# Retention attention and two feed-forward blocks on one core: another form of the warming products, and fewer waits on TensorE in the attention

## The reference

```python
# q, k, v: (4, 8, 768, 64)
for t in range(S):                       # attention with a decaying state
    state = gamma[None, :, None, None] * state + np.einsum('bhd,bhe->bhde', k[:, :, t], v[:, :, t])
    y[:, :, t] = scale * np.einsum('bhd,bhde->bhe', q[:, :, t], state)
...
x = y as (3072, 512)
h = x @ w_in                             # 512 -> 2048
g = np.where(h > 0.0, h, np.exp(np.minimum(h, 0.0)) - 1.0)
x = g @ w_out                            # 2048 -> 512
...
h = x @ w_in2                            # 512 -> 1024
solu = h * softmax(h)
ln = (solu - mean) / sqrt(var + 1e-6) * g_ln
out = ln @ w_out2                        # 1024 -> 512
```

## Time and profile before

| | |
|---|---|
| time, median of 3 runs | 837.15 us (837.04 to 837.56) |
| the profiled execution | 837.55 us, its span 835.8 us |
| TensorE busy | 831.1 us (99% of the span), 4861 product records |
| VectorE, ScalarE, GpSimd busy | 559.2, 412.8, 398.9 us |
| the warming | 13 products from 1.19 us |
| first scores product | 6.50 us |
| first product behind the attention (line 685) | 75.25 us |

### The profile page before, as it was taken

The page is one execution under the profiler, slowest core; times in us unless marked ns, Lnnn a source line. Parts: engine busy times, 40 slices in busy tenths (PEclk is TensorE's granted clock), DMA queues, the critical chain, the costliest instruction groups (busy, mean ns, idle before and its releaser), DMA issues.

```text
span 835.8 us, 12629 instructions
## 1 busy us (share of the span) xinstructions
PE 831.1 (99%) x4861; PEld 692.5 (83%) x4861; DVE 559.2 (67%) x854; ACT 412.8 (49%) x660; POOL 398.9 (48%) x460
## 2 busy tenths in 40 slices
PE   9999999999999999999999999999999999999998
PEld 7998888888888888888888888888888888888886
DVE  5587767678634555575455555788877778777774
ACT  3685766574435555553455555563333343334422
POOL 3797857754026574620267661564334444444200
PEclk9999999999999999999999999999999999999999
DMA  9999312105012010140201001612111111111001
GB/s 351 404 397 320 102 51 69 58 26 177 1 39 63 26 51 26 52 150 1 75 26 51 27 26 54 198 51 76 51 51 51 51 50 39 51 52 51 17 21 51
DMA packets 48651, 72.79 MB, mean 87 GB/s; under 512 B 2896, under 2 KB 23504, under 8 KB 48336
## 3 DMA queue, kind: packets, MB, share of 16 engines
q1 hardware_dynamic: 48448, 71.84, 24.9%
q10 hardware_dynamic: 144, 0.15, 0.1%
HBM read 55.20 MB, written 16.78 MB: 86 GB/s over the span
## 4 chain that ended last, share of the span: by engine, by line
PE 99%; ACT 0%; issue 0%; DVE 0%; ACTq 0%
PE ps L733 10%; PE ps L736 10%; PE ps L732 10%; PE ps L685 9%; PE ps L687 9%; PE ps L686 9%; PE ps L856 5%; PE ps L854 5%; PE ps L855 5%; PE ps L744 5%; PE ps L746 5%; PE ps L745 5%; PE ps L611 3%; PE ps L654 3%; PE ps L840 3%; PE ps L630 1%
## 5 line engine op out<-in xcount | busy, mean ns | idle before, releaser
L523 POOL TENSOR_TENSOR u_lo<-u_raw,u_hi 128x256 fp32r<-128x256 f32 x168 | 141.5, 875 | 192.8 <-ACT u_hi L1250 192.8
L733 PE MATMUL ps<-g_hi,wd_lo 128*128 128x512 f32 x384 | 149.4, 389 | 0.0
L732 PE MATMUL ps<-g_hi,wd_hi 128*128 128x512 f32 x384 | 149.4, 389 | 0.0
L736 PE MATMUL ps<-g_lo,wd_hi 128*128 128x512 f32 x384 | 149.4, 389 | 0.0
L685 PE MATMUL ps<-x_hi,u_hi 128*128 128x512 f32 x336 | 131.3, 391 | 0.0
L687 PE MATMUL ps<-x_lo,u_hi 128*128 128x512 f32 x336 | 130.8, 389 | 0.0
L686 PE MATMUL ps<-x_hi,u_lo 128*128 128x512 f32 x336 | 130.7, 389 | 0.0
L518 POOL TENSOR_TENSOR u_raw<-u_raw 128x256 f32<-128x256 f32 x96 | 88.8, 926 | 16.2 <-DMA u_raw<-w_dram 10.3
L568 POOL TENSOR_TENSOR u_lo<-x_raw,u_hi 128x256 fp32r<-128x256 f32 x84 | 65.5, 814 | 41.8 <-ACT u_hi L1373 41.8
L732 PEld LDWEIGHTS ps<-g_hi,wd_hi 128*128 128x128 f32 x384 | 72.1, 188 | 15.1
L733 PEld LDWEIGHTS ps<-g_hi,wd_lo 128*128 128x128 f32 x384 | 72.1, 188 | 15.0
(11 more groups left out here) (94 smaller groups left out, 1450.4 us busy)
## 6 DMA issues: line engine op xcount, KB each, us to landing
u_raw<-w_dram SPq DMA_DIRECT2D x24, 512.0 KB, 3.5
q<-units_dram SPq DMA_DIRECT2D x12, 512.0 KB, 6.8
k<-units_dram SPq DMA_DIRECT2D x12, 512.0 KB, 8.2
v<-units_dram SPq DMA_DIRECT2D x12, 512.0 KB, 7.9
x_between<-x SPq DMA_DIRECT2D x24, 256.0 KB, 2.8
x_raw<-x_between SPq DMA_DIRECT2D x12, 512.0 KB, 3.6
out_dram<-y_sb SPq DMA_DIRECT2D x24, 256.0 KB, 2.0
kn<-units_dram SPq DMA_DIRECT2D x9, 512.0 KB, 9.7
```

The source lines that it names most:

```text
L523: nc.gpsimd.tensor_tensor(u_lo[n % 2][:, o, :], u_raw[n % 2][:, o, :], u_hi[n % 2][:, o, :].bitcast(f32), ALU.subtract).then_inc(ul_done, 1)
L732: nc.tensor.matmul(ps[:, bank + m, :], hi, g_hi[:, no % 3, :], start=(f == 0), stop=False)
L733: nc.tensor.matmul(ps[:, bank + m, :], lo, g_hi[:, no % 3, :], start=False, stop=False)
L736: last = nc.tensor.matmul(ps[:, bank + m, :], hi, g_lo[:, no % 3, :], start=False, stop=(f == NF1 - 1))
```

## The change

The 13 wide warming products become 3. Behind them come 34 products (17 pairs) of the form of a scores product: 64 rows, 128 columns, float32, lower and upper rows in turn, over a zeroed tile `warm_chunk`, which VectorE clears with a second memset. In `scores` the wait for the mask of the step before is taken out; in `values` the waits for the decayed v are taken out wherever `key_values` of the same step has waited for the same counts.

```diff
-WARM = 13
+WARM, WARM_PAIRS = 3, 17
...
         warm = place("warm", 512, mybir.dt.bfloat16, XH_AT)
+        warm_chunk = place("warm_chunk", 2 * C, f32, XH_AT + 1024)
...
                         pe.wait_ge(q_decayed, 2 * (s - EARLY) + one + 1)
-                    if s > 0:
-
-                        pe.wait_ge(masked, 2 * s - 1 + one)
+
                     q, k = q_sb[slot][:, one, :], k_sb[slot][:, one, :]
...
             def values(s, opens):
                 slot = s % SLOTS
-                pe.wait_ge(v_decayed, s + 1)
-                if s < SHARED:
-                    pe.wait_ge(v_early, s + 1)
+                if s == 0 or s % NC == NC - 1:
+
+                    pe.wait_ge(v_decayed, s + 1)
+                if s == 0:
+                    pe.wait_ge(v_early, 1)
...
             for n in range(WARM):
                 nc.tensor.matmul(ps[:, n % 4, :], warm[:, 0:P], warm[:, :], start=True, stop=True)
+            pe.wait_ge(warm_zeroed, 2)
+            for n in range(WARM_PAIRS):
+
+                for h in (n % HH, HH + n % HH):
+                    nc.tensor.matmul(ps_scores(0, h), warm_chunk[rows(h), 0:C], warm_chunk[rows(h), C:], start=True, stop=True)
...
             nc.vector.memset(warm[:, :], 0.0).then_inc(warm_zeroed, 1)
+            nc.vector.memset(warm_chunk[:, :], 0.0).then_inc(warm_zeroed, 1)
```

## The result

The change makes the kernel slower, by 0.4%. The median is 840.57 us in 12 runs (838.14 to 842.88) against 837.34 us before in 12 runs (836.41 to 838.27): a ratio of 1.0037, 95% interval 1.0027 to 1.0046, or about +3.1 us. The runs also spread over more than twice the width. The prediction's 837.45 is missed, and so is its range, by 0.2 us at the top (840.4). The profiled execution of the changed kernel took 839.59 us (span 837.8), one of the faster ones, 2.0 us over the profiled one of before.

What follows compares the result with a forecast made beforehand. TensorE's own unbroken stream was taken as the bound. Warming +1.5, waits 0 and breaks -1.2 gave +0.3 us on the median of 837.15, so 837.45 us, with a range of 835.7 to 840.4.

Steps and rivals of the forecast that it cites:

- What bounds the kernel: Whole kernel: only TensorE's own stream counts; no other engine's wait ends last in the attention, the part behind keeps its length.
- The warming (+1.5): Start of TensorE's stream: pairs take double time at the low clock, so scores begin at 8.2 us, not 6.5; +1.5 us.
- The waits (0): Scores and values: the 35 removed waits were already met and cost nothing; 0 us, lower bound -0.7.
- The breaks (-1.2): Scores of steps 8 to 11: late instruction packets cost 1.46 us; moved edges would mostly be in time; -1.2 us.
- the breaks stay: Rival, attention: breaks continue at other places, one edge per step, leaving +1.5 us, 838.7 us; chance 0.23.
- late clock: Rival, start: full clock comes later, all 17 pairs slow, +3.7 us, or +2.5 with breaks gone (839.6); chance 0.2.

Runs made afterwards that it cites:

- late_waits: Kernel before with 20 wide warming products instead of 13 and the change's 35 waits taken out: 838.28 us, ratio 1.0013.
- waits_only: Kernel before with its old warming of 13 wide products, only the 35 waits taken out: 836.49 us, ratio 0.9989.
- cols_after: Changed kernel with the loads of q, k, kn and v cut to 256 of 512 columns per chunk from step 3 on: 837.98 us, ratio 1.0010.
- cols_before: Kernel before with the loads of q, k, kn and v cut to 256 of 512 columns per chunk from step 3 on: 836.22 us, ratio 0.9988.
- narrow: Changed kernel with the 34 float32 warming products replaced by 68 bf16 products of 75 columns, as many records: 839.77 us, ratio 1.0029.
- set 3: Kernel before, warming of 3 wide and 42 to 138 narrow products; 64, 128, 192, 256 records more in front: 839.62, 840.32, 838.53, 837.40 us.
- late_start: Kernel before with 20 wide warming products instead of 13, old waits kept: 839.33 us, ratio 1.0027.
- shift128: Kernel before with a warming of 3 wide and 74 narrow products (69 columns), 128 records more in front: 840.32 us, ratio 1.0037.
- half_before: Kernel before with the loads of q, k, kn and v cut to 64 of 128 partitions from step 3 on: 841.64 us, ratio 1.0053.

## Why the prediction was wrong

- **What bounds the kernel**: right. No wait of another engine ends last in the attention after the change, and the stretch behind it has kept its length.
- **The warming (+1.5)**: right in mechanism and size. For a clock at 6.1 us I had the scores at 8.2. In the profiled run it came at 5.4, and the same working gives (5.4 - 2.6)/0.448 = 6.3 slow pairs and 10.7 x 0.224 = 2.4 us, 7.8; measured 7.80. The other profiles with 17 pairs follow the same working: the clock at 6.4, 6.8 and 7.2 us, scores at 8.30, 8.46 and 8.65. What such a start costs at the end is less sure: `late_waits` is 1.2 us slower than the kernel before and 2.0 slower than `waits_only`, with breaks in both figures. Between `cols_after` and `cols_before`, where few breaks are left, there are 1.8 us, of which 0.6 is the one break in the former's profile. The rule of the Trainium skill ("TensorE: Matmul & The Clock Gate", Part 3) that row groups run at once and loads are pulled ahead under them, which I had set aside, would have given an estimated 6.3. At neither clock do the rows of `warm_chunk` agree with both parts of it; which part fails no row here shows.
- **The waits (0)**: right where they stood (step 1's scores still take 1.99 us), incomplete in what they do. As instructions they take part in the supply: `waits_only` gains 0.8 us. My lower bound (-0.7, at 20 ns a wait) did not come from the rows: two waits of 20 ns in a piece would have shown above their 10 ns of rounding.
- **The breaks (-1.2)**: this is the step that failed. I had read rightly what they are (TensorE out of instructions at a packet's edge, the edge moved from mid scores to the seam of values and carried state), and that is where they turned up. But I argued that a packet would mostly be in time there. It was later instead: 2.47 us of breaks in the profiled run instead of the 0.3 that I left. In the median the term is about +1.7 if the start is priced at the 1.5 that I had for it (3.2 in all), so that it was wrong by some 2.9 us. `narrow`, with the change's edges and the old start, is 2.5 us slower by itself, so the two parts do not simply add. My argument looked only at how much work TensorE has queued at the edge. What set 3 shows to count is where the edges fall in a step. Why it counts is argued: the place also sets when in the step's bursts of loads the request for a packet goes out. The profiles of `late_start` and `narrow` suggest that the time at which the stream runs against the transfers counts too, which I had noted and priced at nothing. That the request goes out at the edge before, no record shows; it fits that the next packet starts some 4 us after a break's end in most cases, and within 1.7 us of the edge where the transfers are thin (`cols_before`).
- **The rivals and the range**: "the breaks stay" had the right side with 0.23 and a price that was too small, since I had priced it as if the breaks kept their size. I had named +1.5 as the upper bound of the breaks and then put no case with it into the range; with it, 837.15 + 1.5 + 1.5 = 840.2 would have been an ordinary case and the range's top higher. That the top of 840.4 was missed by only 0.2 is luck, since it stood there for a late clock. A later clock was not the cause: the clock came between 4.3 and 7.2 us in all the profiled runs of the study, with either form of warming.
- Open: why edges in mid values or carried state meet later packets than edges in mid scores, in terms of single transfers; how a later start and the place of the edges act together; and how much of the changed kernel's wider spread comes from the clock's moment and how much from the packets.

## What to carry to other kernels

Where an engine's chain is as dense as TensorE's here, count its instructions per microsecond: at 256 in less than about 6 us, beside full DMA engines, instructions become a resource, and each one put in front or taken out moves where its packets' edges fall. A loss or gain of some tenths of a per cent after an edit of a prologue should be tried again with the stream lengthened by other amounts, a whole packet among them, before it is put down to the edit's own work. Warming is best sized to end before the first data is there. Wide products and pairs alike took twice as long at the low level; 7 pairs cost nothing, and 17 put the first scores product 1.3 us later.

## What was new about the hardware

A long break can be followed by a fall of the clock. In `shift128` the values of step 10 stop for 2.07 us, with 0.98 us of products before and 1.13 behind, and a microsecond later the granted clock is at 0.50 for some 3 us. In stretches (length, PE busy, clock, DMA share, GB/s):

```profile
69.50:72.30 2.80, 0.85 (x15) 1.00 1.13 337
72.40:73.40 1.00, 0.98 (x15) 0.97 1.03 311
73.60:76.60 3.00, 3.00 (x42) 0.50 1.01 300
77.50:80.50 3.00, 3.00 (x70) 1.00 1.10 328
```

The carried state after it takes 1.92 us instead of 1.03 and the next scores 2.61 instead of 1.99. So this break cost 2.07 + 0.89 + 0.62 us, 1.7 times its own length; the run took 843.21 us, the slowest of its five. It need not happen: `half_before` has a wait of 2.13 us for kn that ends at 22.29, and its granted clock stays at 1.00 from 4.8 us on.

```profile
20.00:22.30 2.30, 0.17 (x6) 1.00 1.07 212
22.30:25.00 2.70, 2.70 (x64) 1.00 1.06 207
```
